# Layer two's down projection with the relu block as the stationary operand, its products in another order, and its result scaled by ScalarE in four parts

## The reference

```
logits = x @ w_gate + modality_bias[modality_id]
e_idx = np.argmax(logits, axis=1)
...
for e in range(E):
    mask = e_idx == e
    ...
    h = np.maximum(x[mask] @ w1[e], 0.0)
    out[mask] = gate_w[mask, None] * (h @ w2[e])
```

## Time and profile before

| | |
|---|---|
| median of 3 runs | 1131.33 us (1130.93 to 1133.27) |
| the profiled execution | 1135.07 us |
| its span, first to last instruction | 1133.3 us |
| PE, DVE, ACT, POOL busy | 88%, 67%, 61%, 18% |
| mean granted TensorE clock | 0.95 |
| steps in the loop | 42, each 19.26 us |

### The profile page before, as it was taken

How to read it: one execution, slowest core, us unless ns; L and a number is a source line. 1 busy time by engine, 2 the same in 40 slices (tenths; PEclk the granted TensorE clock), 3 DMA queues, 4 the chain that set the end, 5 groups by cost and what they waited for, 6 DMA issues and landing times.

```text
span 1133.3 us, 28294 instructions
## 1 busy us (share of the span) xinstructions
PE 1001.1 (88%) x6551; PEld 510.2 (45%) x6551; DVE 758.2 (67%) x2211; ACT 686.4 (61%) x1656; POOL 198.7 (18%) x438
## 2 busy tenths in 40 slices
PE   5266446589999999999999999999999999999886
PEld 4144312245445454555455554454554545554342
DVE  3144457566767777777777686767677777777563
ACT  3134346356666676666666666666666766666453
POOL 2691000211111111111111111111111111111000
PEclk9688769699999999999999999999999999999998
DMA  4976665000110101010000010001001010100000
GB/s 129 275 225 218 215 215 172 22 20 28 27 28 19 36 19 32 23 29 26 27 27 27 27 27 27 27 27 27 27 19 35 18 33 22 29 25 20 21 11 20
DMA packets 68615, 64.70 MB, mean 57 GB/s; under 512 B 9570, under 2 KB 60770, under 8 KB 68568
## 3 DMA queue, kind: packets, MB, share of 16 engines
q1 hardware_dynamic: 68568, 64.11, 19.0%
HBM read 40.55 MB, written 23.55 MB: 57 GB/s over the span
## 4 chain that ended last, share of the span: by engine, by line
PE 81%; SPq 6%; DMA 5%; issue 3%; DVE 2%; ACT 2%; POOL 1%; ACTq 0%; DVEq 0%; POOLq 0%
PE y L1224 42%; PE up L1247 22%; PE up L1237 7%; DMA stage<-in_moe_w 2%; SPq L301 2%; DMA GW<-in_x 2%; PE y L1311 2%; SPq L303 2%; PE up L1163 1%; PE TB L1271 1%; PE SM L1295 1%; SPq L316 1%; PE SM L1283 1%; SPq L310 1%; PE TB L1259 1%
## 5 line engine op out<-in xcount | busy, mean ns | idle before, releaser
L811 DVE SCALAR_TENSOR_TENSOR hlo<-up,hhi 128x500 f16<-128x500 f32 x736 | 490.2, 672 | 205.5 <-ACT hhi L560 203.0
L560 ACT ACTIVATE hhi<-up 128x500 f16<-128x500 f32 x736 | 415.5, 586 | 143.3 <-PE up L1237 75.9
L1247 PE MATMUL up<-ytb,W1B 128*128 (+1 forms) x1104 | 277.7, 382 | 17.4 <-issue 14.8
L1224 PE MATMUL y<-hhi,W2A 128*128 128x500 f16 x736 | 217.1, 376 | 1.1 <-DVE hlo L811 1.1
L1224 PE MATMUL y<-hhi,GW 128*128 128x500 f16 x736 | 216.0, 374 | 0.5 <-DVE hlo L811 0.4
L1247 PEld LDWEIGHTS up<-ytb,W1B 128*128 x1104 | 108.6, 99 | 155.8 <-issue 48.2
L1237 PE MATMUL up<-E4T,GW 128*128 (+1 forms) x368 | 138.4, 380 | 0.0
L1224 PE MATMUL y<-hlo,W2A 128*128 128x500 f16 x368 | 137.8, 374 | 0.0
L1224 PE MATMUL y<-hlo,GW 128*128 128x500 f16 x368 | 137.6, 374 | 0.0
L476 POOL TENSOR_TENSOR st<-ss,root 125x4 f32<-125x4 f32 x46 | 46.8, 1018 | 374.5 <-ACT TB L592 374.5
L1224 PEld LDWEIGHTS y<-hhi,W2A 128*128 x736 | 67.8, 97 | 66.6 <-issue 15.5
(11 more groups left out here) (158 smaller groups left out, 1053.5 us busy)
## 6 DMA issues: line engine op xcount, KB each, us to landing
x_turned<-GW SPq DMA_DIRECT2D x46, 250.0 KB, 4.1
xth<-x_turned SPq DMA_DIRECT2D x46, 250.0 KB, 2.6
out<-yout SPq DMA_DIRECT2D x46, 250.0 KB
GW<-in_x SPq DMA_DIRECT2D x46, 240.0 KB
stage<-in_moe_w SPq DMA_DIRECT2D x16, 512.0 KB, 4.2
W1B<-in_moe_w SPq DMA_DIRECT2D x8, 512.0 KB, 7.2
w2s<-in_moe_w SPq DMA_DIRECT2D x8, 512.0 KB, 3.9
GW<-in_x SPq DMA_DIRECT2D x46, 10.0 KB
```

Of the source, the lines that this page charges most:

```text
L560: nc.scalar.activation(hhi[:, (u % UP) * CT:(u % UP + 1) * CT], ups[u % UP][:, 0:CT], ACT.Relu).then_inc(s["hi_done"], 1)
L811: nc.vector.scalar_tensor_tensor(hlo[:, o:o + CT], ups[u % UP][:, 0:CT], 0.0, hhi[:, o:o + CT], ALU.max, ALU.subtract).then_inc(s["lo_done ...
L1224: ins = mm(y[:, 0:CT], W[:, bass.ds(woff + (fb * 2 * C + o), C)], h[:, k * CT:(k + 1) * CT], start=opens and fb == 0 and n == 0, stop=fb = ...
L1247: ins = mm(ups[k][:, 0:CT], W1B[:, bass.ds(woff + (wl * F + fb * P), P)], ytb[:, bass.ds(yoff + yl * CW, CT)], start=n == 0, stop=n == 2)
```

## The change

Of layer two, `down` now takes a 128-point block of `hhi` or `hlo` as the stationary operand and a 128-column block of `W2B` as the moving one: 12 products of 128 columns a unit in place of 3 of 500. The result in `y2` has points on the partitions, so `yt` and `out_transposes` are gone, and so are their semaphores. The two products that read the same columns of `W2B` now stand together. `result` is cut into four parts, one after each of the units 11 to 14 on ACT; the factor 1/`S_OUT`, formerly in `yt`, is in DVE's `factors`. `hhi` and `hlo` get a pitch of `CW` = 504 columns in place of 500, and GpSimd clears their padding once.

```diff
@@ -436,7 +435,7 @@
-            for m in (ytb, E4T):
+            for m in (ytb, E4T, hhi, hlo):
                 nc.gpsimd.memset(m[:, :], 0.0).then_inc(s["pads_cleared"], 1)
...
@@ -597,29 +596,27 @@
-                def yt(after):
-                    act.wait_ge(s["pass_done"], after)
-                    nc.scalar.activation(yT[:, :], y2[:, 0:CT], ACT.Copy, scale=1.0 / S_OUT).then_inc(
-                        s["result_copied"], 1)
...
-                def result():
-                    act.wait_ge(s["gate_steps"], CG * (c + 3))
-                    act.wait_ge(s["out_free"], c + 1)
-                    act.wait_ge(s["result_transposed"], c + 1)
-                    for j in range(TJ):
-                        ins = nc.scalar.activation(yout[:, j * C:(j + 1) * C], y2[0:TQ, j * C:(j + 1) * C], ACT.Copy,
-                                                   scale=coef[:, bass.ds(parity(c) * TJ + j, 1)])
-                    ins.then_inc(s["result_ready"], 1)
+                def result(j, after):
+                    if j == 0:
+                        act.wait_ge(s["gate_steps"], CG * (c + 3))
+                        act.wait_ge(s["out_free"], c + 1)
+                        act.wait_ge(s["pass_done"], after)
+                    ins = nc.scalar.activation(yout[:, j * C:(j + 1) * C], y2[0:TQ, j * C:(j + 1) * C], ACT.Copy,
+                                               scale=coef[:, bass.ds(parity(c) * TJ + j, 1)])
+                    if j == TJ - 1:
+                        ins.then_inc(s["result_ready"], 1)
...
-                            8: [lexps] if rx or ry else [], 10: [lambda: yt(after())] if l2 else [],
-                            13: [exps] if xq else [], 15: [result] if l2 else []}
+                    return {1: [e4t] if rx else [], 4: [squares] if rx else [], 8: [lexps] if rx or ry else [],
+                            11: part(0), 12: part(1), 13: ([exps] if xq else []) + part(2), 14: part(3)}
...
@@ -1216,14 +1214,25 @@
+                def down_by_point(woff, opens):
+                    def down(fb, k):
+                        if fb == 0 and opens:
+                            pe.wait_ge(s["result_ready"], c + 1)
+                        for n, (h, o) in enumerate(((hhi, C), (hhi, 0), (hlo, 0))):
+                            for j in range(TJ):
+                                ins = mm(y2[:, j * C:(j + 1) * C], h[:, k * CW + j * TQ:k * CW + j * TQ + P],
+                                         W2B[:, bass.ds(woff + (fb * 2 * C + o), C)],
+                                         start=opens and fb == 0 and j == 0 and n == 0, stop=fb == NF - 1 and n == 2,
+                                         skip_group_check=True)
                         return ins
                     return down
...
-                def out_transposes():
-                    pe.wait_ge(s["result_copied"], c + 1)
-                    for j in range(TJ):
-                        ins = nc.tensor.transpose(y2[0:TQ, j * C:(j + 1) * C], yT[:, j * TQ:(j + 1) * TQ],
-                                                  ident[:, :])
-                    ins.then_inc(s["result_transposed"], 1)
```

More of the change, by code:

```diff
@@ L92, in attention_two_moe_kernel @@
         E4T = sb("E4T", [P, 2 * CW], f16)[:, :]
-        hhi, hlo = (sb(n, [P, UP * CT], f16)[:, :] for n in ("hhi", "hlo"))
-        yT = sb("yT", [P, CT])[:, :]
+        hhi, hlo = (sb(n, [P, UP * CW], f16)[:, :] for n in ("hhi", "hlo"))
         tmp16 = sb("tmp16", [P, 3, 512], f16)[:, :, :]
@@ L198, in attention_two_moe_kernel @@
             "flag_steps gate_steps "
-            "result_copied result_transposed result_ready out_written out_free ").split()
+            "result_ready out_written out_free ").split()
         names += [f"x_loaded{k}" for k in range(XR_N * STREAMS)] + [f"x_stored{k}" for k in range(XT_N * STREAMS)]
@@ L545, in _ @@
                     nc.scalar.activation(hi, a, ACT.Copy, scale=S_W).then_inc(s["w2b_hi_ready"], 1)
-            act.wait_ge(s["pads_cleared"], 3)
+            act.wait_ge(s["pads_cleared"], 5)
             npas = act.alloc_register("act_pass")
@@ L559, in units @@
                     act.wait_ge(s["up_done"], base + (k + 1))
-                    nc.scalar.activation(hhi[:, (u % UP) * CT:(u % UP + 1) * CT], ups[u % UP][:, 0:CT],
+                    nc.scalar.activation(hhi[:, (u % UP) * CW:(u % UP) * CW + CT], ups[u % UP][:, 0:CT],
                                          ACT.Relu).then_inc(s["hi_done"], 1)
@@ L608, in exps, with part @@
                         s["chunk_exp"], 1)
-                def result():
-                    act.wait_ge(s["gate_steps"], CG * (c + 3))
-                    act.wait_ge(s["out_free"], c + 1)
-                    act.wait_ge(s["result_transposed"], c + 1)
-                    for j in range(TJ):
-                        ins = nc.scalar.activation(yout[:, j * C:(j + 1) * C], y2[0:TQ, j * C:(j + 1) * C], ACT.Copy,
-                                                   scale=coef[:, bass.ds(parity(c) * TJ + j, 1)])
-                    ins.then_inc(s["result_ready"], 1)
+                def result(j, after):
[7 more added lines that the diff above has]
+                        ins.then_inc(s["result_ready"], 1)
                 def tasks(after):
-                    return {1: [e4t] if rx else [], 4: [squares] if rx else [],
-                            8: [lexps] if rx or ry else [], 10: [lambda: yt(after())] if l2 else [],
-                            13: [exps] if xq else [], 15: [result] if l2 else []}
+                    def part(j):
+                        return [lambda: result(j, after())] if l2 else []
+                    return {1: [e4t] if rx else [], 4: [squares] if rx else [], 8: [lexps] if rx or ry else [],
+                            11: part(0), 12: part(1), 13: ([exps] if xq else []) + part(2), 14: part(3)}
                 def step(mixed):
@@ L645, in step @@
                             if l1 and (rx or ry):
-                                tk[14] = [lambda: load_flags(c)]
+                                tk[14] = tk[14] + [lambda: load_flags(c)]
                             units(act.snap(npas, min_val=0, max_val=1 << 20) * NF, range(first, first + n * NF), tk)
@@ L809, in units @@
                     v.wait_ge(s["hi_done"], base + (k + 1))
-                    o = (u % UP) * CT
+                    o = (u % UP) * CW
                     nc.vector.scalar_tensor_tensor(hlo[:, o:o + CT], ups[u % UP][:, 0:CT], 0.0, hhi[:, o:o + CT],
@@ L956, in factors @@
                         hold(v, "result_ready", c + 1)
-                        tell(nc.vector.tensor_tensor(coef[:, now], gs[:, 1, 1, :], c1[:, now], ALU.mult), "gate_steps")
+                        tell(nc.vector.scalar_tensor_tensor(coef[:, now], gs[:, 1, 1, :], 1.0 / S_OUT, c1[:, now], ALU.mult,
+                                                            ALU.mult), "gate_steps")
                     else:
@@ L1217, in pe_step, with down_of @@
                 joint = rx or ry
-                def down_of(W, woff, y, opens, before=None):
+                def down_of(W, woff, y, opens):
                     def down(fb, k):
-                        if fb == 0 and before:
-                            before()
                         for n, (h, o) in enumerate(((hhi, 0), (hhi, C), (hlo, 0))):
-                            ins = mm(y[:, 0:CT], W[:, bass.ds(woff + (fb * 2 * C + o), C)], h[:, k * CT:(k + 1) * CT],
+                            ins = mm(y[:, 0:CT], W[:, bass.ds(woff + (fb * 2 * C + o), C)], h[:, k * CW:k * CW + CT],
                                      start=opens and fb == 0 and n == 0, stop=fb == NF - 1 and n == 2,
                                      skip_group_check=True)
+                        return ins
+                    return down
+                def down_by_point(woff, opens):
[8 more added lines that the diff above has]
+                                         skip_group_check=True)
                         return ins
@@ L1249, in up @@
                         return ins
-                    def before():
-                        pe.wait_ge(s["result_ready"], c + 1)
-                    return up, down_of(W2B, woff, y2, opens, before if opens else None)
+                    return up, down_by_point(woff, opens)
                 def e4():
@@ L1319, in pe_step @@
                 tasks = {1: when(rx, first_router), 2: when(ry, second_router),
-                         7: when(xq, scores), 8: when(joint, counts), 12: when(l2, out_transposes)}
+                         7: when(xq, scores), 8: when(joint, counts)}
                 def step(mixed):
```

## The result

| | before | after |
|---|---|---|
| median | 1131.33 us (1130.93 to 1135.91, 5 runs) | 1140.55 us (1138.46 to 1144.32, 5 runs) |
| profiled execution, its span | 1135.07, 1133.3 | 1140.55, 1138.8 |
| PE, DVE, ACT, POOL busy | 88%, 67%, 61%, 18% | 88%, 67%, 57%, 18% |
| a step of the loop | 19.26 us | 19.37 us |

The changed kernel is slower: ratio 1.0075, 95% interval 1.0047 to 1.0102, which is 5.3 to 11.5 us. A step of the loop is given as nearly all steps take it.

The account below looks back on a forecast made before the run. Took a step to be paced by early downs, DVE's chain to `hlo`(8), PE to up(15), then the sequencer. 0.11 + 0.02 us x 42 = +5.5, last steps -0.2: +5.3 on 1131.33 gives 1136.6 us, range 1125 to 1141.

Parts of the forecast that it names:

- the forecast's own case: Whole kernel: slower by 5.3 us, to 1136.6; its own range +2.5 to +9, 1133.8 to 1140.3; chance 0.60.
- What paces a step: Loop step: early ups and downs to second router, DVE to `hlo`(8), PE to up(15), then relu(15), `hlo`(15), sequencer.
- Downs on the path: Layer two in the loop: three units' downs count, +0.036 us each, +0.11 us a step; the other five cost nothing.
- Transposes off it: Loop, behind down(12): PE loses 0.44 us of transposes a step, which becomes waiting for `hlo`(15); worth nothing.
- The price of a product: Layer two's downs: 0.0555 us per 128-column product, 0.667 us a unit against 0.631.
- Rival 3: PE's downs: weight loads do not hide in long runs, 0.099 us a product, about 1325 us; chance 0.05.
- Its cover: Downs beside DVE's chain: five units' extra 0.18 us goes into PE's waits of 0.13 and 0.14 us.
- The parts on ACT: ACT, units 11 to 14: four result parts delay relu(15), +0.02 us a step; ends 0 and 0.24.
- Rival 1: Step's end: PE is the bound, so the transposes' time is won; 1116 us, half-way 1126.7; chance 0.17.
- Rival 4: PE's loop of 1384 instructions leaves instruction memory, a 3.5 us miss each step, about 1284 us; chance 0.05.
- Together -0.2: Four written-out steps: -1.4 us for `yT` and transposes, +0.4 downs, +0.8 code (ends 0 and 3.5).
- the upper end for the parts: ACT in the loop: 0.24 us a step if a part takes its full 0.37 us; range used half.

Follow-up runs that it names:

- e2: Changed kernel with the downs of units 0 to 2 by points and those of units 3 to 7 in the old form; 1138.14 us (one run).
- e3: Changed kernel with the downs of units 3 to 7 by points and those of units 0 to 2 in the old form; 1138.47 us (one run).
- e1: Kernel before without the copy to yT and the four f32 transposes; 1123.99 us (one run).
- e4: Changed kernel with down(14) waiting for lo_done of unit 14 alone, not unit 15; 1126.43 us, ratio 0.994 to the kernel before.
- e5: Kernel before with down(14) waiting for lo_done of unit 14 alone, not unit 15; 1118.05 us, ratio 0.987.
- e6: Changed kernel with the never-entered branch with masks left out of the four written-out last steps; 1119.97 us.
- e7: Kernel before with the never-entered branch with masks left out of the four written-out last steps; 1115.10 us.

## Why the prediction was right, and where it was off

The forecast was 1136.6 us, the result 1140.55, inside the range of 1125 to 1141 and on the side that was given 0.67, but 0.2 us above 1140.3, where the range of the forecast's own case ended. The change was put at 5.3 us and measured as 9.2 in the medians and 7.5 in the traces. The loop was right by its mechanism. The last steps were not, and that the total still fell inside the range owes something to its width.

- *What paces a step.* Right in each part. Downs on the path: three of eight (e2, e3). Transposes off it (e1). The next step's first up tied to `hlo`(15) by the sequencer (e4; 1.69 us forecast, 1.70 measured). The rise per step was forecast as 0.13 us and is 0.11.
- *The price of a product.* 0.0555 us from four e4 transposes; 0.056 measured over twelve in a row, 0.67 us a down as forecast. The rate of 81 ns that the Trainium skill (TensorE: Matmul & The Clock Gate, Back-to-back issue gap) gives for streams of load and matmul at N = 128 does not occur here: 219 ns rows start 56 ns apart, each with its own load, which is the page's other figure, for a single product's gap. Rival 3 falls.
- *Its cover.* The waits of 0.13 and 0.14 us at down(7) and down(8) went to 0 and 0.09, as the five downs beside DVE's chain needed.
- *The parts on ACT.* Forecast +0.02, measured 0.003 (e3). `exps` handed ACT on after 0.20 us (736.42 to 736.62) where 0.25 was taken, and the part behind it after 0.25 (to 736.87), as taken.
- *Rival 1*, PE the bound at the step's end, is ruled out for both kernels as they were. It comes true once the tie is loosened: in e5 PE's products are what keeps the gain at 0.23.
- *Rival 4*, the longer loop leaving instruction memory, is ruled out: the branch took 208 ns and the step 19.37 us throughout the loop, but for the two steps at its ends, and no instruction transfer falls between 300 and 1000 us.
- *The term that was mis-sized* is the written-out steps: "Together -0.2", with 0.8 for code in it. Measured +2.8. With the code out of the way (e6, e7) the rest of the term is -0.7, where I had put -1.4 + 0.4 = -1.0, so code cost some 3.5 us in place of 0.8. The end of 3.5, "for one more such jump", met that number by luck. The fourth jump did go from 0.36 to 3.29 us, but with the wait of 2.45 behind the short jump it made only 0.9 of it; 2.5 came from a new wait in step 43. e5 agrees: it is the kernel before with a fourth jump of over 3.6 us, and its last steps take 81.2 us, 1.2 less than before, of which its own waits can make 0.7. The prediction took jumps as the only price of code, and left out the waits that come without one and the fall of the clock. So the sum of the loop was good to 0.8 us and the last steps were 3 us short.

```profile
L1365 PEldq COMPARE_BRANCH  x4: 3699/3712/3803, 1032.9 to 1095.3; - x4
```

- The bounds: with the upper end for the parts the loop gives 9.7 us and the total 9.5, where the case's range stopped at 9. And not all steps but the first take 19.26 us; the last takes 22.2.
- The remaining 1.7 us between the traces' 7.5 and the medians' 9.2 was not traced; the kernel before alone had medians up to 1133.90 in later sets.

What stays open: what sets which jumps miss and where a second wait follows. e2 has four jumps over 3.2 us like the changed kernel and still needs 80.1 us for its last steps against 85.2; e1 misses two and needs 72.7. That these steps pay for the code they jump over is shown (e6, e7); the rule by which they do is not. Nor is it shown how much of the +2.8 us another execution of the same two kernels would repeat.

## What to carry to other kernels

A row that is over 99% busy says nothing on which products are on the path: lay out one step by start times, find the few waits of a tenth of a microsecond, and count only the work between them. Count a sequencer's register instructions and branches as work of their own, behind the last wait of a loop's body above all; there a down that waited for the `hlo` of the unit behind its own cost 0.9% of this kernel. Steps written out behind a loop can pay for a branch body that they jump over even if it is never entered: 22 and 19 us here, counting the last step of the loop. Read such steps on their own, with their waits and their clock, and do not price them by the loop's.
